# An RWKV layer whose outputs are laid out in strips, two expert layers behind it, one NeuronCore

## The reference, cut to what matters

```python
# 1. RWKV attention, per batch and head; state is 48 x 48
for t in range(S):
    cur = einsum('bhd,bhe->bhde', u * kt, vt)
    y[:, :, t] = einsum('bhd,bhde->bhe', rt, state + cur)
    state = w * state + einsum('bhd,bhe->bhde', kt, vt)
# 2. dense gated layer: 3072 tokens, 384 -> 1536 -> 384
g = x @ w_gate;  x = (silu(g) * (x @ w_val)) @ w_out
# 3. router over 8 experts (384 -> 1024 -> 384), one expert per token
e_idx = argmax(x @ w_gate2)
out[mask] = gate_w * sigmoid(x @ w_output_gate)[e] * (relu(x @ w1[e]) @ w2[e])
```

## Time and profile before

| | us |
|---|---|
| median of 3 runs | 868.7 |
| lowest, highest | 868.57, 873.98 |
| the profiled execution, its own time | 867.91 |
| its span, first to last instruction | 866.1 |
| PE busy in the span | 839.8 (97%) |
| DVE, ACT, POOL busy | 559.6, 314.8, 173.4 |

### The profile page before, as it was taken

The page is one execution under the profiler, slowest core; times in us unless marked ns, Lnnn a source line. Parts: engine busy times, 40 slices in busy tenths (PEclk is TensorE's granted clock), DMA queues, the critical chain, the costliest instruction groups (busy, mean ns, idle before and its releaser), DMA issues. The chain is left out here.

```text
span 866.1 us, 17077 instructions
## 1 busy us (share of the span) xinstructions
PE 839.8 (97%) x6395; PEld 737.0 (85%) x6395; DVE 559.6 (65%) x1099; ACT 314.8 (36%) x500; POOL 173.4 (20%) x141
## 2 busy tenths in 40 slices
PE   7699999999999999999999999999899999999995
PEld 6578888888888888888788878899899999999995
DVE  8688756674567546644453446469969777887770
ACT  1233233111311131112211321357457766686651
POOL 3633302242133303230101001003020101111010
PEclk9799999999999999999999999999999999999999
DMA  9763430342024302330011002537986668766700
GB/s 360 261 223 135 132 111 9 95 169 66 0 67 146 121 1 66 107 130 1 11 46 38 1 0 72 222 152 246 387 312 243 240 247 322 261 249 248 275 18 18
DMA packets 37283, 125.80 MB, mean 145 GB/s; under 512 B 4236, under 2 KB 21056, under 8 KB 31600
## 3 DMA queue, kind: packets, MB, share of 16 engines
q1 hardware_dynamic: 32848, 108.14, 35.5%
q0 software_dynamic: 3520, 9.87, 3.0%
q10 hardware_dynamic: 864, 7.08, 2.3%
HBM read 107.26 MB, written 18.88 MB: 146 GB/s over the span
## 5 line engine op out<-in xcount | busy, mean ns | idle before, releaser
L1621 PE MATMUL bank<-X1H,WH 128*128 128x512 f32 x432 | 169.0, 391 | 2.5 <-DVE YS L1009 2.2
L1621 PE MATMUL bank<-X1L,WH 128*128 128x512 f32 x432 | 168.2, 389 | 0.0
L1621 PE MATMUL bank<-X1H,WL 128*128 128x512 f32 x432 | 168.2, 389 | 0.0
L808 ACT ACTIVATE SG<-bank 128x512 f32<-128x512 f32 x72 | 43.0, 598 | 231.3 <-PE bank L1621 231.3
L1250 DVE TENSOR_TENSOR TT<-bank,SG 128x512 f32<-128x512 f32 x72 | 49.8, 691 | 115.6 <-ACT SG L808 115.1
L738 ACT ACTIVATE AH<-PP 128x512 fp32r<-128x512 f32 (+1 forms) x78 | 46.1, 598 | 162.3 <-DVE PP L1255 162.3
L1621 PEld LDWEIGHTS bank<-X1H,WH 128*128 128x128 f32 x432 | 81.1, 188 | 21.4 <-issue 4.8
L1621 PEld LDWEIGHTS bank<-X1H,WL 128*128 128x128 f32 x432 | 81.1, 188 | 17.0
L1621 PEld LDWEIGHTS bank<-X1L,WH 128*128 128x128 f32 x432 | 81.1, 188 | 16.3
L1258 DVE TENSOR_TENSOR AL<-PP,AH 128x512 fp32r<-128x512 f32 (+1 forms) x78 | 59.5, 769 | 50.9 <-ACT AH L738 50.9
L1667 PE MATMUL bank<-AH,WH 128*128 128x512 f32 (+1 forms) x234 | 91.4, 390 | 0.0
(11 more groups left out here) (235 smaller groups left out, 1837.5 us busy)
## 6 DMA issues: line engine op xcount, KB each, us to landing
W_EVEN<-w SPq DMA_DIRECT2D x20, 1536.0 KB, 8.4
W_ODD<-w SPq DMA_DIRECT2D x18, 1536.0 KB, 8.2
RK_IN<-unit_rk SPq DMA_DIRECT2D x18, 736.0 KB, 5.5
V_IN<-unit_v SPq DMA_DIRECT2D x18, 448.0 KB, 3.4
STG<-w_dense ACTq DMA_DIRECT2D x6, 1152.0 KB, 6.1
mixed<-YS SPq DMA_DIRECT2D x40, 96.0 KB, 2.3
X<-mixed SPq DMA_DIRECT2D x5, 768.0 KB, 4.3
XG_ODD<-store SPq DMA_DIRECT2D x9, 394.0 KB, 8.4
```

What stands on the lines that cost most here:

```text
L808: nc.scalar.activation(SG[:, :], GATE_PS[:, :], ACT.Sigmoid).then_inc(sig_ready, 1)
L1621: last = mm(bank_[:, :], lhs[:, f, m, k * P:k * P + P], rhs[:, k, :], start=(x == 0), stop=(x == len(terms) - 1))
```

## The change

In the words of the code:
- **Strips.** A pair of heads has 96 channels, three strips of 32; `STRIPS` places the four pairs' strips in the three 128-row tiles of X1. The channels of X1 are in a new order, and the rows of the dense weights with them. `key_sums` and `outputs` write strips of 32 rows (16 matmuls where there were 8, and 32 where there were 16, with tile shapes 64 x 32 and 128 x 32); heads of a pair that share a strip both add to it, with zeros in the other's rows of V and SELU (`VW = 64`). DVE writes the products and sums straight into X1 (`own_key`, `add_output`: four instructions each instead of two). YS, `mixed`, and their DMAs are gone.
- **Start.** Four units instead of six lie ahead of the dense stage; units 4 and 5 move into block 0, so that every block 0 to 4 has four units, 20 in all. Keys of the first units are turned on PE (`turn_keys`) instead of being loaded. The state terms of units 0 to 3 stand behind the first gate and value. The key sums of two units are made together. The first gate takes its terms in the order X1H*WH, X1L*WH, X1H*WL. PE's 30 warm-up transposes of 128 columns become 2 matmuls of 512 columns.
- **Silu in one operation.** ACT writes Silu of the gate into SG; the product by TT is gone (72 DVE instructions). PE waits for `silu_ready` instead of `gate_free`.
- **Route in bank 7.** Logits go to the value bank at f = 0, turned logits and ranks to bank 7 at f = 9 and 10 (in the last block at f = 1 and 2).
- **State.** One scalar_tensor_tensor for each pair does decay and sum (four instructions); the state terms take 16 matmuls in strips instead of 8, in bank 5.
- **Loads.** SP loads unit 4 when the first key sums are done and unit 5 when the first four outputs are; the first dense weights come from SP, ahead of them.
- **Experts.** A tile's first `expert_up` waits for the high weights only in the third early tile, and takes its terms in another order; for the first late tile SP asks for the rows ahead of w2.
- **End.** SP, not POOL, waits for the last scatters.
- PE's loop over blocks 1 and 2 is unrolled.

The diff, cut to what the prediction speaks of:

```diff
+STRIP = 32
+STRIPS = (((0, 0), (0, 2), (0, 1)), ((1, 0), (0, 3), (1, 1)), ((1, 2), (2, 0), (1, 3)), ((2, 2), (2, 1), (2, 3)))
 
...
+class Piece:
+
+
+
+    def __init__(self, h, i):
+        self.head, self.cut = Head(h), slice(STRIP * i, STRIP * i + STRIP)
+        k, strip = STRIPS[h // 2][h % 2 + i]
+        self.out = slice(STRIP * strip, STRIP * strip + STRIP)
+        self.cols = slice(k * P, k * P + P)
+
+
+LOWER = [Piece(h, i) for h, i in ((0, 0), (1, 1), (0, 1), (2, 1), (2, 0), (3, 1), (1, 0), (3, 0))]
+UPPER = [Piece(h, i) for h, i in ((4, 0), (5, 1), (4, 1), (6, 1), (6, 0), (7, 1), (5, 0), (7, 0))]
+BOTH = [p for four in ((LOWER, 0), (UPPER, 0), (LOWER, 4), (UPPER, 4)) for p in four[0][four[1]:four[1] + 4]]
...
+            sp.dma_start(STG[:, :, :, :], w_dense[:, 0:2, :, :]).then_inc(stage_loaded, 16)
+            u4, u5 = units_of_block(0)[0:2]
+            sp.wait_ge(c_ready, 2)
+            sp.nop(nofuse=True)
+            load_unit(u4)
             sp.dma_start(WROUTE[:, :, :], w_route).then_inc(route_loaded, 16)
-            def load_x1_part(b):
-                sp.wait_ge(y_start_stored[b], 32)
-                sp.dma_start(X1[:, :, b * P:b * P + P], mixed_tiles[:, :, b * P:b * P + P]).then_inc(x1_part_loaded[b], 16)
...
-                store_output(u)
+            sp.wait_ge(y_ready, BATCH)
+            sp.nop(nofuse=True)
+            load_unit(u5)
+            sp.wait_ge(dense_low, 3)
+            sp.nop(nofuse=True)
+            sp.dma_start(STG[:, :, :, :], w_dense[:, 2:4, :, :]).then_inc(stage_loaded, 16)
...
             sp.wait_ge(records_sent, 1 + CH)
             sp.wait_ge(pad_written, 16 * NE)
             sp.nop(nofuse=True)
             load_rows_when_free(first, late_row(0))
+            load_w2_when_free(first, e)
             load_tile(second, late_row(1), late_expert(1))
...
+            for tile in END_TILES:
+                sp.wait_ge(out_written[tile.buffer], 16 * (tile.of_buffer + 2))
+            sp.nop(nofuse=True)
...
+                    need(act, value_free, q)
+                    nc.scalar.activation(SG[:, :], GATE_PS[:, :], ACT.Silu).then_inc(silu_ready, 1)
+                    if first and f == 0:
+                        turned_keys(3)
+                        first_state(0)
...
             def own_key(u):
                 u.wait_v(dve)
                 dve.wait_ge(c_ready, u.i + 1)
-                if not u.start:
-                    dve.wait_ge(y_stored[u.odd], 32 * u.nth)
-                for x in range(2):
-                    cols = slice(HALF_COLS * x, HALF_COLS * (x + 1))
-                    last = tt(u.ys[:, cols], u.v[0:PR, I_VT:I_VV][:, cols], u.c_banks[x][0:PR, cols], ALU.mult)
+                if u.first:
+                    last = tt(X1[:, :, u.out], u.v[:, I_VT:I_VV].rearrange("p (k t) -> p k t", k=KT),
+                              u.c[:, 0:DM].rearrange("p (k t) -> p k t", k=KT), ALU.mult)
+                else:
+                    low, high = u.c_banks
+                    tt(X1[LATER, 1, u.out], u.own(1, LATER), high[LATER, P:2 * P], ALU.mult)
+                    tt(X1[:, 2, u.out], u.own(2), high[:, 2 * P:3 * P], ALU.mult).then_inc(gate_sums_used, 1)
+                    tt(X1[:, 0, u.out], u.own(0), low[:, 0:P], ALU.mult)
+                    last = tt(X1[EARLIER, 1, u.out], u.own(1, EARLIER), low[EARLIER, P:2 * P], ALU.mult)
                 last.then_inc(c_used, 1)
...
             def add_state(u):
                 dve.wait_ge(u_ready, u.i + 1)
-                dve.wait_ge(decayed, u.i - BATCH + 1)
-                tt(ST[:, u.b, :, :], u.u[0:PR, 0:PAIRS * HD].rearrange("p (j e) -> p j e", j=PAIRS), ST[:, u.b, :, :],
-                   ALU.add).then_inc(state_ready, 1)
+                dve.wait_ge(state_ready, u.i - BATCH + 1)
+                for s in range(PAIRS):
+                    last = stt(out=ST[:, u.b, s, :], in0=ST[:, u.b, s, :], scalar=WPOW[:, s, 7:8], in1=u.u[0:PR, s * VW:s * VW + VW],
+                               op0=ALU.mult, op1=ALU.add)
+                last.then_inc(state_ready, 1)
...
                     dve.wait_ge(value_ready, q + 1)
-                    dve.wait_ge(gate_free, q + 1)
                     need(dve, act_low, q)
                     def product(part):
-                        return tt(PP[:, part], TT[:, part], VALUE_PS[:, part], ALU.mult)
+                        return tt(PP[:, part], SG[:, part], VALUE_PS[:, part], ALU.mult)
 
...
+            def key_sums(u):
+                pe.wait_ge(rxk_scaled, u.i + 1)
+                pe.wait_ge(c_used, u.i)
+                pe.nop(nofuse=True)
+                opened = set()
+                for p in BOTH:
+                    a, at = p.head, (p.head.x, p.out.start)
+                    last = mm(u.c_banks[a.x][p.out, p.cols], SELU[a.rows, a.s, p.cut], u.rxk[a.rows, a.keys],
+                              start=at not in opened, stop=True, skip_group_check=True)
+                    opened.add(at)
+                last.then_inc(c_ready, 1)
...
+                    for p in BOTH:
+                        a, at = p.head, (p.head.x, p.out.start)
+                        mm(u.y[a.x][p.out, p.cols], ST[a.rows, u.b, a.s, p.cut], u.rw[a.rows, a.keys],
+                           start=at not in opened, stop=False, skip_group_check=True)
+                        opened.add(at)
...
+                for p in LOWER + UPPER:
+                    a = p.head
+                    last = mm((u.y if u.first else u.y[a.x])[p.out, p.cols], u.v[:, a.v:a.v + VW][:, p.cut],
+                              u.am[:, a.x, a.s, :], start=u.first and p.out.start not in opened, stop=True, skip_group_check=True)
+                    opened.add(p.out.start)
...
+                    for strip in range(BATCH):
+                        r, width = STRIP * strip, min(STRIP, PR - STRIP * strip)
+                        v = Head(PAIRS * (strip // 2) + s).v
+                        last = mm(u.u[r:r + width, s * VW:(s + 1) * VW], u.kh[:, s * PR + r:s * PR + r + width],
+                                  u.v[:, v:v + VW], start=True, stop=True)
...
+            for x in range(2):
+                mm(bank[2][:, :], ident, CST[:, C_ID:C_ID + 4 * P], start=True, stop=True)
+            u0, u1, u2, u3 = [Unit(0, b) for b in range(BATCH)]
             scores(u0)
...
+            turn_keys(u0)
+            turn_keys(u1)
...
+            first_key_sums(u0, u1, False)
+            first_key_sums(u0, u1, True)
             outputs(u0)
-            key_sums(u0, CROSSED)
-            key_sums(u1, STRAIGHT)
+            scores(u2)
             outputs(u1)
-            key_sums(u1, CROSSED)
-            scores(u2)
-            state_terms(u0)
-            key_sums(u2, STRAIGHT)
-            state_terms(u1)
-            key_sums(u2, CROSSED)
             scores(u3)
+            turn_keys(u2)
+            first_key_sums(u2, u3, False)
+            first_key_sums(u2, u3, True)
             outputs(u2)
-            key_sums(u3, STRAIGHT)
-            state_terms(u2)
-            key_sums(u3, CROSSED)
             outputs(u3)
-            state_terms(u3)
-            key_sums(u4, STRAIGHT)
-            scores(u4)
-            key_sums(u4, CROSSED)
-            outputs(u4)
-            state_terms(u4)
-            key_sums(u5, STRAIGHT)
-            scores(u5)
-            key_sums(u5, CROSSED)
...
                 terms = [(lhs, rhs, k) for k in range(KT) for lhs, rhs in ((WH, X1H), (WH, X1L), (WL, X1H))]
+                opening = isinstance(n, int) and n == 0 and m == 0 and f == 0
+                if opening:
+                    terms = sorted(terms, key=lambda t: (t[1] is X1L) + 2 * (t[0] is WL))
+                    pe.wait_ge(x1_high, KT)
                 for x, (lhs, rhs, k) in enumerate(terms):
-                    if x % 3 == 0 and m == 0 and f == 0:
+                    if opening and x == KT:
+                        pe.wait_ge(x1_low, KT)
+                    if opening and x == 2 * KT:
+                        pe.wait_ge(dense_low, 1)
+                    if x % 3 == 0 and m == 0 and f == 0 and not opening:
                         pe.wait_ge(x1_low, KT * n + k + 1)
...
+                        for k in range(KT):
+                            mm(to, wh[:, w[k]], XH[:, k, :], start=(k == 0), stop=False)
+                        if weights_late:
+                            pe.wait_ge(x_low, tile.after)
+                            for k in range(KT):
+                                mm(to, wh[:, w[k]], XL[:, k, :], start=False, stop=False)
+                            for k in range(KT):
+                                pe.wait_ge(w1_low, 3 * tile.n + k + 1)
+                                last = mm(to, wl[:, w[k]], XH[:, k, :], start=False, stop=(k == KT - 1))
...
                         if f == 0:
                             turn(n)
-                        if f == 1:
-                            pe.wait_ge(gate_free, q + 1)
+                            pe.wait_ge(value_free, q + 1)
```

(6 more changed lines are left out.)

656 lines of the change are left out of this document (306 added, 350 removed).

## The result

The changed kernel took 859.08 us (median of 4 runs, 855.71 to 859.61), the kernel before 870.49 in the same session. The ratio is 0.9856, with a 95% interval of 0.9811 to 0.9901: faster, by less than 2%. The forecast was 857.7, range 851 to 867. The profiled execution took 859.41 us, 8.5 less than that of before; the forecast's sum was 11.0. Six more runs of the same file later gave 856.31 us (855.44 to 859.50) against 873.82 for the kernel before, ratio 0.982 (0.9792 to 0.9849).

A forecast was written before the change was run, and what follows sets the result against it. PE, with work in flight 97% of the span, was taken to bound the kernel. Terms of -16.5, +8.4, +2.9, +0.3, -1.9, -2.6 and -1.6 sum to -11.0 us: 857.7 us from the median, range 851 to 867.

The forecast's parts named there:

- Start, forecast -16.5: Before the dense stage: first dense matmul moves from 41.98 to an effective 25.5 us, saving 16.5 us.
- first line of the ledger: Stretch from the start to the first turning transpose in block 1: forecast change -15.2 us.
- second case of the forecast: Start: more DVE-PE waits or dense work at 1.2 GHz give back 5.5 to 7.5 us, about 864; chance 0.20.
- Work moved, strips and routing behind it, forecast +8.3: Turning in block 1 to first row transpose: two more units (7.9), 16 units of strips, and routing; +8.3 us.
- routing: Blocks 1 to 4, second gate no longer late, and last block, wait for LG gone: -1.9 us.
- Strips, forecast +2.9: Units' small matmuls: parallel rounds stay 109 ns; shape changes add 2.0 us and wider state terms 0.9.
- rival of a floor: Key sums, state outputs and state terms: small passes cost 27 ns each, +22.9 us, 881 us; chance 0.12.
- Block 0's stalls, forecast 1.7: Block 0: unit 4's scores 0.8 us late, second gate 0.85 us late; together 1.7, net change +0.3.
- Silu 0: Dense stage: dropping 72 DVE operations of 0.69 us changes nothing, since no PE wait there is theirs.
- loads 0: Later loads of units 4 and 5 and RK_IN cost nothing, unless a queue of over 8 us precedes RK_IN.
- Experts, forecast -2.6: Expert stage: waits at the third early tile (0.78) and first late tile's rows (1.57) go; -2.6 us.
- End -1.6: After the last scatter: 4.8 us of closing work can start at POOL's last issue; -1.6 us, bounds 0 and -4.6.

The follow-up runs named there:

- first trace: Profiled execution of the changed kernel, no further edit, with two stretches at the lower clock: 859.41 us.
- second trace: Profile from later unedited runs of the changed kernel, at mean clock 0.998; those six runs took 856.31 us.
- undone kernel: Changed kernel with the expert edits undone and the last wait back on POOL instead of SP: 864.62 us, ratio 0.9932.

## Why the prediction was right, and where only its sum was

**Start, forecast -16.5: right but for the clock.** The dense stage was to begin as if at 25.5. In the first trace its first matmul starts at 23.60 and loses 1.32 in the wait for X1L, which is as if at 24.9; in the second trace 24.47 and 1.07, 25.5. That the second fits so well is partly luck. I had put 1.5 us for the lower clock at the very start, where the first trace lost none (its scores ran at the full clock from 9.34 on) and the second 0.8; the relay of engines was longer by 1.2 and 1.0 instead. In the first trace 1.1 of that is an X1L part costed at 0.5 us, which took 1.63 behind POOL's product. What failed is where the lower clock would fall. I had left dense work to a rival; it fell on dense matmuls of block 0 and cost 4.2 there, nearly the whole of the missing 4.5. In the second trace, without such a stretch, the first line of the ledger reads -14.3 instead of -10.7, with -15.2 forecast. So the second case of the forecast (start given back in part) came true in 5 of 10 runs, going by their mean clocks, by one of the two mechanisms it named, dense work at 1.2 GHz, at less than its price of 5.5 to 7.5.

**Work moved, strips and routing behind it, forecast +8.3: +9.1.** With two units at 3.95 (7.9) and 16 units of strips at the 0.17 measured (2.7), 1.5 is left for routing, where 1.9 was forecast. Of these 0.79 lie in the last block (62.12 us from turning to the first row transpose instead of 62.91), where 0.7 was forecast. The early release of the gate bank is worth 2.5 us in blocks 1 to 4, but the wait it saves there was only 0.20 a block before, because two products released it instead of four.

**Strips, forecast +2.9: right mechanism, a little more.** A unit grew by 0.17 us (key sums 0.12, scores 0.04, state terms 0.02), 3.4 over 20 units. The rounds stayed at four per 32 passes, and the group pays about 0.11 once. The key sums' 0.60 is above the 0.44 to 0.50 set down as a sign, by this change of shape, which the sum carried in a term of its own. The rival of a floor is dead: a pass costs 18.7 ns as a mean over the group and 15.3 at the margin, both under the 20 from which it would have decided. The Trainium skill's page "TensorE: Matmul & The Clock Gate" ("Wait — 56ns, not 53.3ns?") has 25 ns as the least distance between starts; for passes to different tiles the trace does not agree.

**Block 0's stalls, forecast 1.7: 2.2.** Both stood where they were put, 0.69 before unit 4's scores and 1.50 before the second gate. The second was 0.65 longer than forecast, since AL, 0.69 us alone, took 1.63: it ended 0.55 behind a POOL product, as in eleven more traces.

**Silu 0, loads 0: right**, Silu to the hundredth.

**Experts, forecast -2.6, measured -5.3: a wait that the sum lacked.** The waits of 0.78 and 1.57 went as forecast: from the third early tile's row transposes to those of the first late tile (601.29 to 621.26, now 599.71 to 617.23) it is 2.45 less. What was missed is a wait that no bracket shows. PE where a half tile's `down` ends and the next pair tile's `up` begins, and DVE's last low rows (XL), before:

```profile
657.05 0.55 DVE L1220 TENSOR_TENSOR XL<-bank,XH 128x384 fp32r<-128x384 f32 x1
...
657.31 0.34 PE L1720 MATMUL bank<-W2H_EVEN,HL 128*128 128x384 f32 x1
657.73 0.38 PE L1699 MATMUL bank<-XH,W1H_ODD 128*128 128x256 f32 x1
657.94 0.28 PE L1700 MATMUL bank<-XL,W1H_ODD 128*128 128x256 f32 x1
658.06 0.28 PE L1701 MATMUL bank<-XH,W1L_ODD 128*128 128x256 f32 x1
```

and after:

```profile
653.24 0.33 PE L1739 MATMUL bank<-W2H_EVEN,HL 128*128 128x384 f32 x1
653.42 0.50 PE L1707 MATMUL bank<-XH,W1H_ODD 128*128 128x256 f32 x3
```

From start to start 0.42 before and 0.18 after: a wait of 0.24 for the low rows, ready at 657.59, covered by the 0.34 for which the last matmul's record runs on. With the first two matmuls of `up`, 0.21 apart instead of 0.11, it is some 0.35 us a tile (0.66 at the first), seven such tiles, 2.8 us by their row transposes. The new order of terms (both high and low weights with XH first, XL last, and the wait for XL behind them) took it away. The undone kernel kept that order and has the 0.18 in every tile; no run puts the old order back by itself.

**End -1.6: right**, 4.8 us behind POOL's last issue in both traces with the wait on SP. With the wait on POOL it is 6.4 in the kernel before and in the undone one.

## What to carry to other kernels

Sum a stretch by fixed marks from start to start: a wait shorter than the record of the matmul before it has no bracket, and seven such waits were worth more than the two that had one. Where a relay of engines leaves PE waits of a microsecond, fill them with work that is due later anyway: together with DVE's products made earlier and POOL's made later it brought block 1 forward by 3.7 us (124.91 to 121.23), and no run showed the clock loss that half of the changed kernel's had. And when a DVE step looks slow, look at what POOL does in the same microsecond: here the two ran in turn, so moving one only chose who waited.
